# Gathered rows turned by VectorE and carried through the parking transfer with h, in place of TensorE's transposes

## What is computed

```python
for e in range(E):                      # first layer: N, D, E, F = 3072, 512, 8, 1024
    for k in range(2):
        mask = top2[:, k] == e
        h = np.maximum(x[mask] @ w1[e], 0.0)
        out[mask] += top2_w[mask, k, None] * (h @ w2[e])
...
for e in range(E):                      # second layer, on the first one's output
    mask = expert_idx == e
    h = np.maximum(xe @ w1[e], 0.0)
    out[mask] = gate_w[mask, None] * (h @ w2[e])
```

## Time and profile before

| | us |
|---|---|
| runs of the kernel before (three) | 1163.91, 1166.44, 1166.90; median 1166.44 |
| the profiled execution | 1165.77 |
| its span in the profile | 1163.7 |
| TensorE (matmul) busy | 1083.5, 93% |
| VectorE busy | 643.8, 55% |
| ScalarE busy | 280.2, 24% |
| GpSimd busy | 315.2, 27% |

### The profile page before, as it was taken

One profiled execution on the slowest core, in us unless ns is written; L12 is line 12 of the kernel. 1 busy time (PEld: TensorE's weight loads), 2 busy tenths in 40 slices (PEclk: granted clock), 3 DMA queues, 4 the chain that ended last, 5 costly groups with the idle time before them and its releaser, 6 DMA issues.

```text
span 1163.7 us, 29685 instructions
## 1 busy us (share of the span) xinstructions
PE 1083.5 (93%) x7939; PEld 877.4 (75%) x7940; DVE 643.8 (55%) x1360; ACT 280.2 (24%) x534; POOL 315.2 (27%) x473
## 2 busy tenths in 40 slices
PE   5888787999999999999999999989889999999994
PEld 4766576788888888888888888855668887878783
DVE  2768585555553552644636446317875346576860
ACT  3566311121221212122121212214211212121211
POOL 2004313322222232322323332211133222333321
PEclk8889798999999999999999999999999999999998
DMA  8999964877685675866857666557387447777951
GB/s 342 352 323 312 334 220 147 224 216 214 187 238 140 208 209 140 235 190 164 239 162 217 199 164 190 147 124 219 116 256 235 147 156 229 236 244 231 311 175 61
DMA packets 126991, 245.87 MB, mean 211 GB/s; under 512 B 17455, under 2 KB 70879, under 8 KB 126961
## 3 DMA queue, kind: packets, MB, share of 16 engines
q1 hardware_dynamic: 48608, 112.38, 29.4%
q10 hardware_dynamic: 61728, 90.25, 24.4%
q0 software_dynamic: 16624, 42.88, 16.9%
HBM read 169.51 MB, written 76.73 MB: 212 GB/s over the span
## 4 chain that ended last, share of the span: by engine, by line
PE 68%; DMA 11%; DVE 8%; issue 5%; ACT 3%; DVEq 3%; ACTq 1%; SPq 0%; POOL 0%; POOLq 0%
PE moe_ps_h L1597 10%; PE moe_ps_y L1597 10%; PE moe_ps_y L1599 10%; PE moe_ps_h L1599 10%; PE moe_ps_h L1598 10%; PE moe_ps_y L1598 10%; DMA moe_h_moved<-h_d 4%; DMA h_d<-moe_h_turned 2%; PE moe_ps_x L1590 2%; DMA k_sb<-in_k 2%; DVE weights L141 2%; PE ps_s L680 1%; ACT pr L883 1%; DVEq L1478 1%; ACTq L1657 1%
## 5 line engine op out<-in xcount | busy, mean ns | idle before, releaser
L1597 PE MATMUL moe_ps_h<-weights,moe_x_hi 128*128 (+1 forms) x640 | 252.5, 395 | 16.4 <-DVE moe_x_lo L1687 16.4
L1597 PE MATMUL moe_ps_y<-weights,moe_h_hi 128*128 (+1 forms) x624 | 251.4, 403 | 10.6 <-DVE moe_h_lo L1707 7.7
L1599 PE MATMUL moe_ps_h<-weights,moe_x_lo 128*128 (+1 forms) x640 | 250.7, 392 | 0.0
L1598 PE MATMUL moe_ps_h<-weights,moe_x_hi 128*128 (+1 forms) x640 | 250.6, 392 | 0.0
L1599 PE MATMUL moe_ps_y<-weights,moe_h_lo 128*128 (+1 forms) x624 | 245.0, 393 | 0.0
L1598 PE MATMUL moe_ps_y<-weights,moe_h_hi 128*128 (+1 forms) x624 | 244.3, 391 | 0.0
L1707 DVE SCALAR_TENSOR_TENSOR moe_h_lo<-moe_h_moved,moe_h_hi 128x256 fp32r<-128x256 f32 x312 | 111.6, 420 | 233.4 <-ACT moe_h_hi L1671 233.4
L1671 ACT ACTIVATE moe_h_hi<-moe_h_moved 128x1024 fp32r<-128x1024 f32 x78 | 82.7, 1061 | 384.6 <-PE moe_ps_y L1599 313.9
L147 DVE TENSOR_TENSOR weights<-stage,weights (+1 forms) x128 | 156.8, 1225 | 19.7 <-DVE weights L141 19.7
L1597 PEld LDWEIGHTS moe_ps_h<-weights,moe_x_hi 128*128 128x128 f32 x640 | 121.0, 189 | 47.8 <-issue 16.7
L1597 PEld LDWEIGHTS moe_ps_y<-weights,moe_h_hi 128*128 128x128 f32 x624 | 118.1, 189 | 35.1 <-issue 7.0
(11 more groups left out here) (259 smaller groups left out, 853.9 us busy)
## 6 DMA issues: line engine op xcount, KB each, us to landing
stage<-in_w SPq DMA_DIRECT2D x128, 512.0 KB, 4.6
h_d<-moe_h_turned ACTq DMA_DIRECT2D x80, 512.0 KB, 4.1
moe_h_moved<-h_d ACTq DMA_DIRECT2D x320, 128.0 KB
v_sb<-in_v SPq DMA_DIRECT2D x24, 520.0 KB, 5.5
k_sb<-in_k SPq DMA_DIRECT2D x24, 512.0 KB, 6.2
x_d<-zero SPq DMA_DIRECT2D x27, 260.0 KB, 5.2
q_sb<-in_q SPq DMA_DIRECT2D x24, 256.0 KB, 4.6
x_d<-x_sb ACTq DMA_DIRECT2D x24, 256.0 KB, 5.9
```

The source lines that it names most:

```text
L1597: pe.matmul(out, a_hi, b_hi, start=(i == 0), stop=False)
L1598: pe.matmul(out, a_hi, b_lo, start=False, stop=False)
L1599: mm = pe.matmul(out, a_lo, b_hi, start=False, stop=(i == len(parts) - 1))
```

## The change

TensorE transposes the gathered rows of the first tiles only (0 to 4 of the first layer, 0 to 3 of the second). For all later tiles VectorE turns the 32x32 blocks of the gathered rows (`turn_x(t+3)`, four instructions, ahead of `turn(t+1)` in turn t), they stand beside h in a common tile `turned` (12 blocks of 32 columns for each quarter, 8 of h and 4 of x), and `park(t+1)` and `fetch(t+1)` carry h of tile t+1 and x of tile t+3 together: 768 KB each where there were 512. `high_x` and `low_x` read x from `moved` in SBUF instead of PSUM. `turn` uses two transposes a half instead of one. GpSimd gathers one tile further ahead (t+6 in a loop that is shifted by one), scatters ahead of the gather, and uses `xg_b` for one more tile of each layer's start and tile 1 of the first layer. The first turn of each loop is written out ahead of it.

```diff
     def park(self, act, t, with_x=False):
         act.wait_ge(s("turned"), t * 2 + 4)
+        if with_x:
+            act.wait_ge(s("xt_done"), t + 3)
         if not (isinstance(t, int) and t == 0):
             act.wait_ge(s("moved"), t * (16 * QB))
-        act.dma_start(self.h_d, self.h_turned[:, :, :, :].rearrange("p b c q -> p (b c q)")).then_inc(s("parked"), 16)
+        n = TC if with_x else FC
+        act.dma_start(self.parts[:, :, 0:n * QR], self.turned[:, :, 0:n, :].rearrange("p b c q -> p b (c q)"))\
+           .then_inc(s("parked"), 16)
...
+        if with_x:
+            act.wait_ge(s("x_split"), t + 2)
+        n = TC if with_x else FC
         for b in range(QB):
-            act.dma_start(self.h_moved[b * QR:(b + 1) * QR, :, :, :].rearrange("p a c q -> p a (c q)"),
-                          self.h_blocks[b]).then_inc(s("moved"), 16)
+            act.dma_start(self.moved[b * QR:(b + 1) * QR, :, 0:n, :].rearrange("p a c q -> p a (c q)"),
+                          self.blocks[b][:, :, 0:n * QR]).then_inc(s("moved"), 16)
...
+    def high_x(self, act, t, moved=False):
+        if moved:
+            act.wait_ge(s("moved"), t * (16 * QB) - 16 * QB)
+            act.wait_ge(s("l1_done"), t * 2)
+            act.nop(nofuse=True)
+            act.activation(self.x_hi[:, :, :].rearrange("p c (a q) -> p c a q", a=QB),
+                           self.moved[:, :, FC:TC, :].rearrange("p a c q -> p c a q"), ACT.Copy)\
+               .then_inc(s("x_high"), 1)
...
+    def turn_x(self, dve, t, second=False):
+        s, xg = self.s, self.xg_b if second else self.xg
+        if second:
+            dve.wait_ge(s("gathered_b"), 32)
+        else:
+            dve.wait_ge(s("gathered"), t * 16 - 16)
+        dve.wait_ge(s("parked"), t * 16 - 32)
+        dve.nop(nofuse=True)
+        for cc in range(DC):
+            last = dve.transpose(self.turned[:, :, FC + cc, :],
+                                 xg[:, cc * P:(cc + 1) * P].rearrange("p (b q) -> p b q", b=QB))
+        last.then_inc(s("xt_done"), 1)
...
     def vector_loop(self, dve, begin, m):
             self.splits(dve, frm, mid)
+            if not first and not end:
+                self.turn_x(dve, t + 3)
             self.turn(dve, t + 1)
-            self.low_x(dve, t + 2)
+            if not end:
+                self.low_x(dve, t + 2, moved=not first)
+            if first:
+                self.turn_x(dve, t + 3, second=True)
             self.splits(dve, mid, to)
             self.low_h(dve, t, end)
...
     def tensor_loop(self, pe, begin, m):
         with pe.Fori(begin, m + 1) as t:
             self.first_product(pe, t + 1)
-            self.x_transposes(pe, t + 2)
             self.second_product(pe, t - 1)
...
+    def pool_loop(self, pool, m):
+        with pool.Fori(1, m) as t:
+            self.scatter(pool, t)
+            pool.wait_ge(s("xt_done"), t + (LAG + 1))
             pool.nop(nofuse=True)
-            self.keep_gate(pool, t + 3)
-            self.gather(pool, t + 4)
-            self.scatter(pool, t)
+            self.keep_gate(pool, t + LAG)
+            self.gather(pool, t + (LAG + 1))
```

The opening of the first layer on GpSimd, with the second buffer:

```diff
             x.gather(pool, 0)
-            for t in range(1, EARLY):
-                pool.wait_ge(s("xt_done"), t)
-                x.keep_gate(pool, t - 1)
-                x.gather(pool, t)
+            x.gather(pool, 1, second=True)
+            pool.wait_ge(s("xt_done"), 1)
+            x.keep_gate(pool, 0)
+            x.gather(pool, 2)
+            pool.wait_ge(s("xt_done"), 2)
+            x.keep_gate(pool, 1, second=True)
```

More of the change, by code:

```diff
@@ L625, in _ @@
             x.scatter(pool, 0)
-            m = x.tiles(pool)
-            pool.wait_ge(s("xt_done"), EARLY + 1)
-            x.keep_gate(pool, EARLY)
-            x.gather(pool, EARLY + 1)
-            x.pool_loop(pool, 1, m)
+            m = x.gathered_ahead(pool)
+            pool.wait_ge(s("xt_done"), 4)
+            x.keep_gate(pool, 3)
+            x.gather(pool, 4)
+            x.gather(pool, 5, second=True)
+            pool.wait_ge(s("xt_done"), 5)
+            x.keep_gate(pool, 4)
+            x.gather(pool, 6)
+            pool.wait_ge(s("gathered_b"), 32)
+            x.keep_gate(pool, 5, second=True)
+            x.pool_loop(pool, m)
             pool.sem_inc(sem("x2_whole"), 1)
@@ L805, in _ @@
             ranks(2, NT)
-            x.x_transposes(pe, 1)
+            x.x_transposes(pe, 1, second=True)
             x.first_product(pe, 1)
@@ L1436, in __init__ @@
         self.early_rows = ((AT[2] if routes.k == 2 else AT2[1]) + 1) * P
-        self.gathers = 16 if routes.k == 2 else 0
-        self.h_blocks = h_d.rearrange("(a p) (b r) -> b p a r", a=QB, b=QB)
+        self.parts = h_d.rearrange("p (b r) -> p b r", b=QB)
+        self.blocks = h_d.rearrange("(a p) (b r) -> b p a r", a=QB, b=QB)
         if same is not None:
-            self.x_hi, self.x_lo, self.h_turned, self.h_moved = same.x_hi, same.x_lo, same.h_turned, same.h_moved
+            self.x_hi, self.x_lo, self.turned, self.moved = same.x_hi, same.x_lo, same.turned, same.moved
             self.h_hi, self.h_lo, self.h_hi_end, self.h_lo_end = same.h_hi, same.h_lo, same.h_hi_end, same.h_lo_end
@@ L1481, in tiles, with gathered_ahead @@
         return self.table(eng, self.routes.full, 0, self.routes.least - 2, self.routes.tiles - 2)
+    def gathered_ahead(self, pool):
+        return self.table(pool, self.routes.full, 1, self.routes.least + 1 - LAG, self.routes.tiles + 1 - LAG)
     def load_piece(self, sp, e, j):
@@ L1556, in keep_gate @@
         else:
-            at = self.xg[:, bass.ds(self.table(pool, self.routes.expert, t, DM, DM + E - 1), 1)]
+            at = (self.xg_b if second else self.xg)[:, bass.ds(self.table(pool, self.routes.expert, t, DM, DM + E - 1), 1)]
         pool.tensor_copy(self.routes.gate[:, bass.ds(t, 1)], at).then_inc(self.s("gated"), 1)
@@ L1587, in x_transposes @@
         else:
-            pe.wait_ge(self.s("gathered"), t * 16 + (16 if isinstance(t, int) and t == 0 else self.gathers))
+            pe.wait_ge(self.s("gathered"), max(t, 1) * 16)
         for cc in range(DC):
@@ L1683, in weigh, with low_x @@
            .then_inc(s("y_ready"), 1)
-    def low_x(self, dve, t):
+    def low_x(self, dve, t, moved=False):
         dve.wait_ge(self.s("x_high"), t + 1)
-        dve.tensor_tensor(self.x_lo[:, :, :], self.ps_x[:, :, :], self.x_hi[:, :, :].bitcast(F32), ALU.subtract)\
-           .then_inc(self.s("x_split"), 1)
+        if moved:
+            last = dve.tensor_tensor(self.x_lo[:, :, :].rearrange("p c (a q) -> p c a q", a=QB),
+                                     self.moved[:, :, FC:TC, :].rearrange("p a c q -> p c a q"),
+                                     self.x_hi[:, :, :].bitcast(F32).rearrange("p c (a q) -> p c a q", a=QB),
+                                     ALU.subtract)
+        else:
+            last = dve.tensor_tensor(self.x_lo[:, :, :], self.ps_x[:, :, :], self.x_hi[:, :, :].bitcast(F32),
+                                     ALU.subtract)
+        last.then_inc(self.s("x_split"), 1)
     def turn(self, dve, t):
@@ L1697, in turn @@
             dve.nop(nofuse=True)
-            dve.transpose(self.h_turned[:, 2 * f:2 * f + 2, :, :].rearrange("p b c q -> p (b c q)"),
-                          self.ps_h[:, f, :]).then_inc(s("turned"), 1)
+            for b in range(2):
+                last = dve.transpose(self.turned[:, 2 * f + b, 0:FC, :].rearrange("p c q -> p (c q)"),
+                                     self.ps_h[:, f, b * (FC * QR):(b + 1) * (FC * QR)])
+            last.then_inc(s("turned"), 1)
+    def turn_x(self, dve, t, second=False):
+        s, xg = self.s, self.xg_b if second else self.xg
+        if second:
+            dve.wait_ge(s("gathered_b"), 32)
+        else:
+            dve.wait_ge(s("gathered"), t * 16 - 16)
[5 more added lines that the diff above has]
+        last.then_inc(s("xt_done"), 1)
     def low_h(self, dve, t, end=False):
@@ L1725, in vector_loop, with tile @@
         s, before, middle = self.s, self.routes.before, self.routes.middle
-        def tile(t, end=False):
+        def tile(t, first=False, end=False):
             frm, mid, to = self.counts(dve, t, (before, t), (middle, t), (before, t + 1))
@@ L1753, in scalar_loop, with tile @@
     def scalar_loop(self, act, begin, m):
-        def tile(t, end=False):
-            self.high_x(act, t + 2)
-            self.park(act, t + 1)
+        def tile(t, first=False, end=False):
+            if not end:
+                self.high_x(act, t + 2, moved=not first)
+            self.park(act, t + 1, with_x=not end)
             self.high_h(act, t, end=end)
             self.weigh(act, t - 1)
-            self.fetch(act, t + 1)
-        with act.Fori(begin, m) as t:
+            self.fetch(act, t + 1, with_x=not end)
+        tile(begin, first=True)
+        with act.Fori(begin + 1, m) as t:
             tile(t)
```

53 lines of the change are left out of this document (30 added, 23 removed).

## The result

The changed kernel takes 1278.97 us (median of four, 1273.03 to 1285.45), beside 1165.18 of the kernel before in the same comparison: 1.097 times as long (95% interval 1.093 to 1.101), so slower by some 114 us. The direction was as forecast. The size was not: 40 us had been forecast, and the time lies above the range, where rival C stood. The profiled execution took 1282.46 us, its span is 1280.8.

A forecast was written before the change was run, and what follows sets the result against it. TensorE was taken to bound the first loop and nearly the second. +25 us in the first loop, +16 in the second and -1 in the opening made +40: 1165.8 became 1205.8, said as 1205, range 1160 to 1260.

The forecast's parts named there:

- rival C: Both loops: each transfer grows by 1.2 us or more; +74 and +39 us, 1278 in all; chance 0.12.
- What bounds the kernel, and the spare: TensorE bounds the first loop, nearly the second; the fetch of h lands with 2.6 us to spare.
- VectorE's work: Each tile: four added transposes 0.8 us, with issue and split turn 1.15; costs nothing in tiles without splits.
- What it moves, and this decides: Loops: high_x now waits for the fetch's landing, low_x for high_x, closing three circles from fetch to fetch.
- split turn's circle: First loop, two splits behind low_x: 13.4 us from fetch to fetch, in 15 of 48 tiles.
- What it adds to the transfers: Park and fetch each grow by 0.26 MB, 0.6 us: fetch 5.9 to 6.5, park 3.4 to 4.0.
- Plain turns: First loop, turns with no split behind low_x: 11.2 us from fetch to fetch, set for 33 tiles.
- The second loop: 12 split turns of 14.3 us, seven tiles of 9.6, four of 10.9: 282.4 against 266, +16.
- The opening: Ahead of the loops: second tile's gather no longer waits for the first tile's transposes; 1 us less.
- A: TensorE stays the bound, waits covered, transposes' time given back: 1132 us, or up to 1155; chance 0.12.
- B: About even: transfers hardly grow; first loop 544 us, second 0 to +8, 1162 to 1174 in all; chance 0.14.
- Its sign: In the loops, TensorE as much idle in turns without splits as in the others would show rival C.

The follow-up runs named there:

- e12: Kernel before with four added transposes of 128 columns a tile on VectorE, into a spare tile nobody reads: 1174.76 us, ratio 1.006.
- e2: Kernel before, with high_x in the loops also waiting for the landing of h, transfers still 512 KB: 1213.72 us, ratio 1.036.
- e1: Kernel before with parks and fetches of 768 KB, the added blocks being zeros nobody reads: 1196.79 us, ratio 1.026.
- e6: Changed kernel with all but the first four weight pieces loaded only to a quarter of their columns: 1262.36 us, ratio 1.083.
- e5: Kernel before with both 768 KB transfers and high_x waiting for the fetch, x still turned on TensorE: 1278.15 us, ratio 1.096.
- e7: Changed kernel with x in its own park and fetches, issued ahead of the park of h, h back at 512 KB: 1372.36 us, ratio 1.178.

## Why the prediction was right in direction and wrong in size

**What bounds the kernel, and the spare.** Right. TensorE bounded the first loop, and with one transpose in place of four it gave 17 us there (forecast by the same term: 48 x 0.35 = 17). In the second loop it gave nothing; the prediction had TensorE nearly the bound there.

**VectorE's work.** By itself: 0.88 us for the four transposes, for 0.8 set; nothing in the first loop (e12), 6.8 us in the second, where split turns grew by 0.73 (12.79 to 13.52) for the 1.15 set. Right, a little high.

**What it moves, and this decides.** Right in mechanism. The wait for the landing made the circles (e2: split turns 13.40 us for 11.38). That e2 has just the 13.4 of the forecast is chance: its fetch landed after 5.92 us, 0.6 less than the term had, and from `low_x` to `low_h` it took 5.12 us, 0.6 more. In the changed kernel the split turn's circle is 7.19 for the landing, 0.17 to `high_x`, 0.66 to `low_x`, 4.83 to `low_h`, 1.6 to the next fetch: 14.45, for the 13.4 set. So two thirds of the miss of 1.05 are the transfer. 15 x 1.05 = 16 us.

**What it adds to the transfers: the step that failed.** A fetch was to go from 5.9 to 6.5 us and a park from 3.4 to 4.0. The parks were set too high (3.64 in the first loop), the fetches far too low there: 7.38. Two errors are in it. The added 0.26 MB cost 1.19 us in the first loop's mean, and 0.96 in e1, about twice the 0.6 set, while the engines' own time for them grew just by the bytes:

```profile
q10 hardware_dynamic: 34560, 75.51, 38.7%
```

That is 3.21 us a MB in 627 us, for 3.16 of the earlier trace rows. The 0.6 was argued from the engines' rate, and no kind of turn of the first loop shows a growth so small; in the second loop it was 0.49 in the mean (5.97 to 6.46). The Trainium skill (DMA: Bandwidth & Descriptors, section "Anatomy of one DMA") has its rate for DMAs that GpSimd issues; the estimate from it for this term was 0.60 us. The trace does not agree in the first loop, for DMAs that ScalarE issues, with 0.79 us in plain turns, 1.20 in split ones and 1.58 in following ones. And the base of 5.9 was read from a plain turn and used for 33 turns. Fourteen of these are following turns, whose fetch took 6.83 us in the kernel before already, and whose fetch and park together, 6.85 + 4.18 = 11.03 us, left but 0.46 of their turn. That was there to be read. After: 8.82 + 3.74 + 0.2 = 12.76 us, not 11.2: 14 x 1.56 = 22 us. That the weight loads make their fetch late, e6 shows.

**Plain turns.** 12.06 for 11.2, 18 x 0.86 = 15 us. Their transfers would let them go at 7.12 + 3.73 + 0.2 = 11.05; what they wait for is TensorE (in all 18 `high_h` was released by `moe_ps_y`). That it is late from the turns ahead, and at times at half clock, fits the rows of the clock above; how much is which is open. The prediction named the clock as a thing without a row and left it out. With the one turn of 14.85 these are 16 + 22 + 15 + 4 = 57 us, the whole gap between 25 forecast and 81.5 measured.

**The second loop.** Split turns 14.40 for 14.3: the number is right, and that is luck. The sum, 13.1 + 1.15, priced VectorE alone, and both its terms were too high: split turns took 12.79 before, and with VectorE's work alone 13.52 (e12). The landing, which the sum left out here, makes the rest: e5, with wait and size and without that work, has 14.33. The eleven others took 10.81 each for a mean of 10.1: 8 us, less catching up than thought. The forecast's 266 us for the loop before was 3 short of the 269.1 between the same fetches. So +22.6 for +16.

**The opening.** -1 forecast; 2.9 us more measured. The kernels with the changed gathers took 42.1 to 44.6 there (e7 49.6), the others 40.2 to 41.8: some 2 us of real cost. Nothing was tried to find its cause.

**The rivals.** A fell with the profile and with e5. B fell with e2: with transfers that do not grow at all, the wait alone costs the first loop 30 us. C had the time (1278) and the growth of the first loop's fetches, 1.2 us; its price for turns without splits behind `low_x`, 12.4, lies between the 12.06 and 12.76 measured, and its 14.0 for split ones was 0.45 short. But it let parks grow as much, and they grew by 0.16, and its two loops, +74 and +39, were +81.5 and +22.6: the hit in the total is in part luck. Its sign, as much idle in turns without splits as in the others, can't tell it from the forecast, since the idle time that a split turn makes stands in the next one. It was given 0.12, because the growth was priced near the engines' time alone.

## What to carry to other kernels

Before bytes are hung on a transfer that is nearly on the path, read its landing for each kind of turn, the worst above all, and what else uses the DMA engines then: here the added bytes cost 1.58 us in the worst turns, where the engines' rate gave 0.82. A read of data that moves from an early source to a landing brings with it everything queued behind it on its engine; look for each circle that this closes. And a queue that works in order must not come to a wait for a transfer that it has only just issued: one call, moved behind other work, was worth 188 us here. A total that comes out right is not yet a mechanism: the second loop's turn of 14.3 and rival C's 1278 were both sums of errors that cancelled.

## What the runs showed of the hardware that was not expected

- Four transposes of 128x128 float32 on VectorE in a row take 0.88 us, and two of 256 columns (VectorE's row of the changed kernel, below) 0.74, hardly more than one of 512, 0.72 us.

```profile
502.81 0.74 DVE L1745 STREAM_TRANSPOSE moe_turned<-moe_ps_h 128x256 f32<-128x256 f32 x2
```

- Half as many bytes again on a transfer of four DMAs: in the first loop 0.8 us more in turns without weight pieces, 1.6 where pieces of 512 KB were in the air; in the second 0.3 and 0.7.
- Two costs that alone were 1 and 30 us in a loop were 67 together, as the first had just fitted under TensorE's turn and no longer did with the second.
- The granted clock fell to 1.2 GHz behind waits of TensorE like the one of 5.81 us above; the split and following turns, whose end TensorE did not set, stayed as long when it came back (14.47 for 14.45, 12.68 for 12.76).
